# Half-slot moves of the attention visits, and products of zeros in pieces of 128 columns

## What is computed

```python
for t in range(S):
    kt, vt, rt, wt = (k[:, :, t], v[:, :, t], r[:, :, t], w[:, :, t])
    cur = np.einsum('bhd,bhe->bhde', u[None] * kt, vt)
    y[:, :, t] = np.einsum('bhd,bhde->bhe', rt, state + cur)
    state = wt[:, :, :, None] * state + np.einsum('bhd,bhe->bhde', kt, vt)
...
x = attn_out.transpose(0, 2, 1, 3).reshape(B * S, H * D)     # 3072 tokens x 384
h = x @ w_in;  x = (max(h, 0) + alpha * min(h, 0)) @ w_out   # 384 -> 2048 -> 384
h = x @ w_in2; x = (h * clip(h + 3, 0, 6) / 6) @ w_out2
```

## Time and profile before

| | us |
|---|---|
| median of 3 runs | 961.78 |
| lowest, highest | 960.14, 962.85 |
| the profiled execution | 963.65 |
| its span (first to last instruction) | 961.7 |
| TensorE busy | 938.2 |
| VectorE busy | 590.8 |
| ScalarE busy | 317.0 |

### The profile page before, as it was taken

One profiled execution on the slowest core, in us unless ns is written; L12 is line 12 of the kernel. 1 busy time (PEld: TensorE's weight loads), 2 busy tenths in 40 slices (PEclk: granted clock), 3 DMA queues, 4 the chain that ended last, 5 costly groups with the idle time before them and its releaser, 6 DMA issues.

```text
span 961.7 us, 23774 instructions
## 1 busy us (share of the span) xinstructions
PE 938.2 (98%) x10708; PEld 784.9 (82%) x10708; DVE 590.8 (61%) x894; ACT 317.0 (33%) x628; POOL 50.4 (5%) x38
## 2 busy tenths in 40 slices
PE   6979999999999999999999999999999999999998
PEld 5879888888888888888888888888888888888886
DVE  6776958755775686397448994544445445445443
ACT  4655453334253534423433321222122212112211
POOL 0000000000000000000006860000000000000000
PEclk7999999999999999999999999999999999999999
DMA  6952071043005202500005330010010100000000
GB/s 177 273 163 75 4 210 51 3 140 88 35 22 153 88 3 67 161 35 2 3 1 197 99 132 1 1 66 0 1 66 1 35 32 0 33 1 1 33 1 33
DMA packets 18740, 59.75 MB, mean 62 GB/s; under 512 B 2416, under 2 KB 2672, under 8 KB 18640
## 3 DMA queue, kind: packets, MB, share of 16 engines
q1 hardware_dynamic: 18640, 58.25, 20.4%
HBM read 48.80 MB, written 9.44 MB: 61 GB/s over the span
## 4 chain that ended last, share of the span: by engine, by line
PE 84%; DVE 2%; issue 1%; ACT 1%; DVEq 0%
PE banks L1041 38%; PE banks L1026 37%; PE banks L904 4%; PE banks L972 1%; PE banks L956 1%; PE banks L917 1%; PE banks L984 1%; PE banks L931 1%; DVE S L702 0%; DVE S L704 0%; DVE pos L768 0%; DVE A L666 0%; ACT Yt L488 0%; ACT pos L529 0%; DVE gh L772 0%
## 5 line engine op out<-in xcount | busy, mean ns | idle before, releaser
L1041 PE MATMUL banks<-gh,wsp 128*128 128x512 f32 (+1 forms) x1248 | 397.7, 376 | 0.9 <-DVE y2T L810 0.9
L1041 PEld LDWEIGHTS banks<-gh,wsp 128*128 128x128 f32 x1248 | 230.3, 188 | 44.5 <-issue 1.8
L1041 PE MATMUL banks<-gl,wsp 128*128 128x512 f32 (+1 forms) x624 | 232.8, 373 | 1.0 <-issue 1.0
L784 DVE SCALAR_TENSOR_TENSOR pos<-pos,banks 128x512 f32<-128x512 f32 x96 | 66.0, 688 | 175.2 <-ACT pos L538 175.2
L538 ACT ACTIVATE pos<-banks,three 128x512 f32<-128x512 f32 x96 | 66.2, 690 | 284.0 <-PE banks L1026 284.0
L1026 PE MATMUL banks<-xh_even,wsp 128*128 128x512 f32 (+1 forms) x672 | 153.7, 364 | 0.4 <-ACT xh_even L494 0.3
L768 DVE SCALAR_TENSOR_TENSOR pos<-neg,minus_slopes,pos 128x512 f32<-128x512 f32 (+1 forms) x112 | 86.2, 770 | 109.2 <-ACT pos L529 108.7
L1026 PE MATMUL banks<-xh_odd,wsp 128*128 128x512 f32 x576 | 148.5, 393 | 0.1
L1041 PEld LDWEIGHTS banks<-gl,wsp 128*128 128x128 f32 x624 | 117.6, 188 | 19.6
L1026 PEld LDWEIGHTS banks<-xh_even,wsp 128*128 128x128 f32 x672 | 114.0, 188 | 20.5 <-ACT xh_even L494 0.9
L1026 PEld LDWEIGHTS banks<-xh_odd,wsp 128*128 128x128 f32 x576 | 106.8, 188 | 22.7 <-issue 0.6
(11 more groups left out here) (71 smaller groups left out, 650.7 us busy)
## 6 DMA issues: line engine op xcount, KB each, us to landing
stage<-in_w_dram SPq DMA_DIRECT2D x32, 384.0 KB, 5.2
K<-in_k_dram SPq DMA_DIRECT2D x12, 448.0 KB, 3.8
W<-in_w_dram SPq DMA_DIRECT2D x12, 448.0 KB, 4.4
R<-in_r_dram SPq DMA_DIRECT2D x12, 448.0 KB, 7.6
KU<-in_k_dram SPq DMA_DIRECT2D x11, 448.0 KB, 4.3
A<-in_r_dram SPq DMA_DIRECT2D x11, 448.0 KB, 6.3
V<-in_v_dram SPq DMA_DIRECT2D x12, 384.0 KB, 7.4
xin<-x_dram SPq DMA_DIRECT2D x6, 768.0 KB, 5.9
```

What stands on the lines that cost most here:

```text
L784: nc.vector.scalar_tensor_tensor(out=pos[:, j], in0=pos[:, j], scalar=6.0, in1=psum[i % HR], op0=ALU.min, op1=ALU.mult).then_inc(g_ready, 1)
L1041: last = nc.tensor.matmul(psum[YBANK + window][:, 0:n], w_[a][:, window * 128:(window + 1) * 128], g_[b], start=(f == 0 and j == 0), stop= ...
```

## The change

```diff
     IDLE = (1792, 0, 0, 0, 0, 0, 256, 0, 0, 0, 384)
-    AT_FIRST = (0, 4, 7, 10, 13, 14, 15, 16, 18, 20)
-    AT_SECOND = (-8, -6, 0, 4, 8, 11, 13, 14, 15, 16, 19, 21, 22, 24, 25)
-    AT_STEP = (-5, -4, 0, 5, 7, 10, 12, 14, 15, 16, 18, 19, 21, 23, 25)
+    AT_FIRST = (0, 4, 7, 10, 13, 15, 16, 17, 19, 21)
+    AT_SECOND = (-8, -6, 0, 4, 8, 11, 13, 15, 16, 17, 18, 20, 22, 23, 25)
+    AT_STEP = (-5, -4, 0, 5, 7, 10, 12, 14, 15, 16, 18, 20, 22, 23, 25)
...
-                    for at in range(0, columns, U):
-                        n = min(U, columns - at)
+                    for at in range(0, columns, 128):
+                        n = min(128, columns - at)
```

## The result

| | us |
|---|---|
| changed kernel, median of 7 runs | 967.1 (965.22 to 971.79) |
| kernel before, beside it, median of 7 runs | 962.4 (958.65 to 967.09) |
| ratio | 1.0051, 95% interval 1.0034 to 1.0067 |
| profiled execution of the changed kernel | 965.22 (span 963.3), the fastest of its seven |

The change costs 4.9 us (3.3 to 6.4); forecast was +1.7. The two profiled executions lie only 1.57 us apart, so most of what is missing is in no row of this pair. That is the puzzle of this case: first the pair, then what other executions do.

The account below looks back on a forecast made before the run. TensorE, busy 938.2 of 961.7 us, was the bound. Zeros +0.0, blocks to 60 us +1.3, step 0 -0.6, its block +0.5, step 1 +1.4, steps 2 to 4 -0.9: +1.7, giving 963.5 us (960.0 to 967.0).

Parts of the forecast that it names:

- the level 2 stop: TensorE's second instruction stop before 60 us, forecast to move to the end of level 2's visit; VectorE stands 3.8 us.

## What to carry to other kernels

When instructions are added or taken anywhere, mark every later block boundary in the list and look for those that bracket a run of quick instructions. Here blocks with 1.7 to 3.4 us of work could stop the engine with no load under way, some in one execution and not in the next; beside loads longer ones did too. Where a kernel's stops differ from one execution to the next, take at least two profiles of each version and compare stretch by stretch; the stretches with steady times carry terms that the total can't show. A visit moved on TensorE moves its copy on ScalarE's list too, and what stands behind that copy decides what the move costs.

## What the runs showed of the chip that was not expected

- A block of instructions that held 1.8 us of work was followed by the next only after 2.49 and 2.9 us, at a DMA share of 0.00.
- 85 of 89 idle times that the timelines put down to "issue" ended 2.2 to 3.05 us after the start of a packet of the instruction queue.
- The stop at one and the same boundary was 0 in one execution of a kernel and 1.67 us in another; the level 2 stop ranged from none to 3.84 us. Another, at 119.41 us in the changed kernel, was 0.75 or 0.76 us in four executions.
- Of seven idle times of 1.6 to 1.8 us on TensorE behind 60 us (waits and stops alike), four were followed within 0.3 to 1.2 us by a granted clock of 0.50 (1.2 GHz) and three were not. Where the hidden layer ran in it, it cost 1.5 us. Before 60 us, nine of the seventeen profiles have such a fall, for 3.4 or 6.8 us.
